# One full tile of the fullest expert worked off between a fused attention/MoE kernel's dense part and its routed loop

## The chip, the cores and the metric

The kernel runs on one core of a Trainium2 chip. The metric is device time in microseconds (us): the time before is the median of 3 runs, and one more execution was taken with the hardware profiler. The core's engines, as the profile names them: PE (TensorE, its weight loads as PEld), DVE (VectorE), ACT (ScalarE), POOL (GpSimd) and SP (SyncE, which here only issues transfers; POOL issues some too).

## The reference

Three stages, all in float32:

```python
kv = einsum('bhsd,bhse->bhde', k, v); out = einsum('bhsd,bhde->bhse', q, kv)      # linear attention, 4 x 8 x 576 x 64
x = rms_norm(out) * g_norm                                                       # then 2304 tokens x 512
# dense mixture: every token through each of 4 experts, weighted by p
for e in range(4): out += p[:, e:e+1] * (maximum(x @ w1[e], 0) @ w2[e])          # 512 -> 1024 -> 512
# routed mixture: each token through one of 8 experts, the best by cosine with expert_emb / tau
for e in range(8): out[idx == e] = gate[idx == e] * (maximum(x[idx == e] @ w1[e], 0) @ w2[e])
```

With the inputs used, the eight routed experts get 120, 639, 189, 727, 149, 36, 293 and 151 tokens, which is 1, 5, 2, 6, 2, 1, 3 and 2 tiles of up to 128 rows: 22 tiles. Of the first 1536 tokens expert 3 gets 484, more than any other.

## The kernel before

Every float32 product is made of three matmuls over operands split into a high and a low part (`three`): high x high, low x high, high x low. ACT makes the high part, DVE or POOL the low one.

**Dense part.** Tokens are worked in thirds of 768 (6 tiles of 128); each third runs 16 steps, 48 in all (k = 0 to 47, `LAST` = 47). A step is `up` (seven block products, written into four PSUM banks and combined by DVE in `combine`) and then `down` for the six tiles of the step before, each added into its rows by a DVE `add` (L965). DVE's list for a step is `combine(k)` and then the six adds; in late steps it also splits the routed experts' weights ahead of time (L973), which SP stores to the DRAM tensor `split_parts`. The last twelve downs stand in an order written out by hand (`TAIL`), with the routing of the last six tiles between them: `flip` (transposes, L1355), `logits` (L1370), `ranks` (L1383 to L1387) on PE; argmax, ranks and slots on DVE; norms on POOL. Blocks of two or three tiles are routed at a time; the first 1536 tokens (12 tiles) are routed and written to their rows by step 38, the last 768 in the tail.

**Dispatch.** POOL's `scatter` (L548) writes each token's row to the DRAM tensor `dispatched_rows`, where each expert has a region. After the last block DVE works out tables of the tiles (L1100 to L1140): which row each tile starts at (`table_row_of_tile`, semaphore `tab_ready` 1), which place in the order of experts it has (`table_place_of_tile`, `tab_ready` 2), and what SP needs to load weights (`tab_ready` 3). A last, partly filled tile of an expert starts further back, and rows that repeat are not stored twice.

**Routed loop.** Tile n: `flip_rows` transposes its rows (L1432), ACT and DVE split them (`rx`, L816 and L1146), `routed_up` makes 24 matmuls, ACT takes the ReLU, `flip_hidden` transposes the hidden rows (L1466), ACT and DVE split them (`rt_parts`, L826 and L1158), `routed_down` makes 24 matmuls, DVE scales by the gate, POOL stores (L608) and loads the rows of a later tile (L594). PE works on up(n+1) before down(n). An expert's split weights are eight pieces of 1 MiB, four for up and four for down; SBUF has two slots, and SP loads the next expert's weights into one while the other is read. A slot's up half is free once the last up of its expert is done, its down half after the last down.

**Between the two.** SP loads the up weights of experts 0 and 1 (L352, eight pieces) once the dense ups are done, then waits for `tab_ready` 1 and all 18 scatters, copies the rows of tiles 0 and 1 (L410), waits until both are there, and loads the down weights of both (L352, eight pieces). The slots of the down weights lie on the dense part's buffers, so they can't be filled before it ends. `load_first` keeps two pieces under way: each waits for the landing of the one before the last. PE runs 48, 8 and 12 matmuls on a unit matrix (L1484, L1487, L1491), whose results nobody reads.

Of the kernel before, what the change touches and what calls it, by code (L numbers as in the profile page):

```python
# [5 lines left out]
F32 = mybir.dt.float32  # L6
# [9 lines left out]
def build(nc, q, k, v, g_norm, probs, w1a, w2a, emb, tau, w1b, w2b, out):  # L16
# [47 lines left out]
    ROUTE_AT = {0: 18, 1: 20, 2: 34, 3: 36}  # L64
    AHEAD_AT = list(range(2, 15)) + [20] + list(range(22, 31)) + [36] + list(range(38, 46))
# [120 lines left out]
    two = keep("two_first", [P, E2])  # L186

# [8 lines left out]
    with ExitStack() as ctx:  # L196
# [28 lines left out]
        filled, scattered = sem("filled"), sem("scattered")  # L225

        part_in = [[sem(f"routed_w{m}_in{c}") for c in range(2)] for m in (1, 2)]
        first_rows_in = [sem("first_rows_in0"), sem("first_rows_in1")]
# [70 lines left out]
        def _(sp):  # L299
# [45 lines left out]
            def load_first(n):  # L345

                e, m, c = n // PCS % 2, n // (2 * PCS), n % PCS
                if n >= 2:

                    e_, m_, c_ = (n - 2) // PCS % 2, (n - 2) // (2 * PCS), (n - 2) % PCS  # L350
                    sp.wait_ge(part_in[m_][c_ % 2], 16 * (e_ * PCS // 2 + c_ // 2 + 1))
                sp.dma_start(W[:, n * PIECE:(n + 1) * PIECE].bitcast(F32),  # L352
                             parts[e, :, (m * PCS + c) * PIECE:(m * PCS + c + 1) * PIECE]).then_inc(part_in[m][c % 2], 16)
# [54 lines left out]
            sp.wait_ge(scattered, 16 * TT)  # L408
            for s in range(2):
                sp.dma_start(xs[:, s, :], rows[bass.ds(first_rows[s], P), :]).then_inc(first_rows_in[s], 16)  # L410

            for s in range(2):
# [24 lines left out]
        def _(pool):  # L437
# [102 lines left out]
            def scatter(b):  # L540

                if b == 0:
                    pool.wait_ge(filled, 32)
                pool.wait_ge(ids_made, BLOCKS[b][0] // TPT + 1)
                pool.wait_ge(slots_ready, b + 1)
                pool.wait_ge(gate_done, b + 1)
                for t in range(*BLOCKS[b]):
                    g.indirect_dma_start(out=rows, out_offset=bass.IndirectOffsetOnAxis(ap=slots[:, t:t + 1], axis=0),  # L548
                                         in_=acc[:, t, :], in_offset=None).then_inc(scattered, 16)
# [40 lines left out]
            pool.wait_ge(scattered, 16 * TT)  # L590

            def load_rows(kk, s):
                r = pool.value_load(tab_r[0:1, bass.ds(kk, 1)], min_val=0, max_val=E2 * CAP + P)
                pool.dma_start(xs[:, s, :], rows[bass.ds(r, P), :]).then_inc(rows_in[s], 16)  # L594


            for s in range(2):

                pool.wait_ge(rx_done, s + 1)
                pool.wait_ge(gi_copied, s + 1)  # L600
                load_rows(s + 2, s)
# [10 lines left out]
            with pool.Fori(0, PAIRS) as i:  # L612
# [13 lines left out]
        def _(act):  # L626
# [179 lines left out]
            for t in range(TT - TPT, TT):  # L806
# [4 lines left out]
            exponentials(NB - 1)  # L811


            def rx(n, s):
                act.wait_ge(rx_done, n + 1)
                A(rxh[:, s, :], ps[:, 7 * s, :], ACT.Copy).then_inc(rx_hi, 1)  # L816

            def relu_rows(n):
                for half in range(2):
                    act.wait_ge(rh_done, 2 * n + half + 2)  # L820
                    A(hs[:, half * 512:(half + 1) * 512], ps[:, 1 + half, :], ACT.Relu).then_inc(rh_relu, 1)

            def rt_parts(n, s):
                for half in range(2):
                    act.wait_ge(rt_done, 2 * n + half + 1)
                    A(rhh[:, s, half * 512:(half + 1) * 512], ps[:, 3 + half, :], ACT.Copy).then_inc(rt_hi, 1)  # L826


            for s in range(2):
                act.wait_ge(s_out[s], 32 * (NAHEAD // 2))  # L830
            act.wait_ge(tab_ready, 2)
            tiles = act.value_load(tab_n[0:1, 0:1], min_val=TT, max_val=KT)
            rx(0, 0)
            rx(1, 1)
            relu_rows(0)
            rt_parts(0, 0)
            with act.Fori(0, PAIRS) as i:
# [16 lines left out]
        def _(dve):  # L854
# [190 lines left out]

            for k in range(STEPS):
                t = k // NU
                if k % NU == 0 and k:
# [23 lines left out]
            for n, (kk, j) in enumerate(TAIL):  # L1072
                add(kk, j)
                if n == 7:
# [30 lines left out]
            step(V.tensor_scalar(ec(5), ec(1), float(-P), float(CAP), ALU.mult, ALU.add), False)  # L1105
# [14 lines left out]
            step(V.scalar_tensor_tensor(kc_(5), kc_(3), float(P), kc_(0), ALU.mult, ALU.add))  # L1120
# [5 lines left out]
            step(V.tensor_copy(tab_n[:, 0:1], ec(2)[:, E2 - 1:E2]), False)  # L1126
# [13 lines left out]
            V.tensor_copy(tab_c[:, :], ec(8)).then_inc(tab_ready, 1)  # L1140
            dve.wait_ge(tab_ready, 3)


            def rx(n, s):
                dve.wait_ge(rx_hi, n + 1)
# [396 lines left out]
```

## Time and profile before

| | us |
|---|---|
| median of 3 runs | 1151.87 (1150.92 to 1154.58) |
| the profiled execution's own time | 1151.53 |
| span of its profile | 1149.9 |

| engine | busy, share of the span |
|---|---|
| PE | 1125.5 us, 98% |
| DVE | 728.5 us, 63% |
| POOL | 655.9 us, 57% |
| ACT | 455.3 us, 40% |

Some 1.6 us of the execution's time lie outside the span. PE is busy nearly always, but part of what it does in the middle is the unread matmuls, so its busy share is not its useful share. All times in rows below are microseconds from the span's start; a mean or a duration is given in ns where a column says so.

### The profile page before, as it was taken

To read this page: it belongs to the slowest core of one execution; us is meant where nothing else is said; L and a number is where in the kernel's file an instruction comes from. 1 tells how busy PE (TensorE), PEld (TensorE's weight loads), DVE (VectorE), ACT (ScalarE), POOL (GpSimd) and SP (SyncE) were. 2 spreads that over 40 slices of the span, in tenths; PEclk is the share of its full clock that TensorE was granted. 3 is DMA by queue.
4 is the path that set the end of the run, shared out by engine and by line. 5 is a ranking of instruction groups with operands and counts; after the bars stand their busy time and mean duration, and the time that the engine had idled before them with its cause. 6 is when DMAs were issued, how large, how long until landed. Compare 5 with 4: busy or idle time off the path is not lost.

```text
span 1149.9 us, 18699 instructions
## 1 busy us (share of the span) xinstructions
PE 1125.5 (98%) x6206; PEld 992.3 (86%) x6207; DVE 728.5 (63%) x1159; ACT 455.3 (40%) x808; POOL 655.9 (57%) x609
## 2 busy tenths in 40 slices
PE   8999999999999999999999999999999999999996
PEld 8888889999889888998889888998887788888885
DVE  4877888888976788888875878888662222222221
ACT  4773444444434444444434444444222222222220
POOL 1587777799867777899867777777330111111101
PEclk9999999999999999999999999999989999999998
DMA  9955777777512448877612448777369749427960
GB/s 245 268 157 180 267 268 271 278 275 276 199 45 78 142 131 302 289 278 261 216 37 75 137 146 302 279 273 270 144 243 383 273 183 372 153 100 302 374 238 13
DMA packets 102433, 250.87 MB, mean 218 GB/s; under 512 B 8254, under 2 KB 48190, under 8 KB 94171
## 3 DMA queue, kind: packets, MB, share of 16 engines
q1 hardware_dynamic: 97360, 235.18, 59.2%
q0 software_dynamic: 4800, 14.72, 3.7%
q8 instruction: 41, 0.67, 0.2%
q14 instruction: 29, 0.24, 0.1%
q10 hardware_dynamic: 203, 0.05, 0.0%
HBM read 170.99 MB, written 79.98 MB: 218 GB/s over the span
## 4 chain that ended last, share of the span: by engine, by line
PE 82%; DVE 7%; POOL 4%; issue 3%; DMA 2%; ACT 2%; SPq 0%; DVEq 0%; POOLq 0%; ACTq 0%
PE ps L1277 25%; PE ps L1279 25%; PE ps L1278 25%; PE ps L1466 2%; DMA w_raw<-in_moe_w_dram 1%; DVE x_rows L965 1%; POOL w_lo L483 1%; PE ps L1235 1%; PE ps L1432 1%; PE ps L1370 1%; DVE hT_lo L954 1%; PE ps L1205 1%; DVE attn_rows L887 1%; DVE x_ops_lo L978 1%; DVE hT_lo L952 0%
## 5 line engine op out<-in xcount | busy, mean ns | idle before, releaser
L1277 PE MATMUL ps<-x_ops_hi,w_hi 128*128 128x384 f32 x672 | 226.5, 337 | 3.4 <-DVE sum L935 3.2
L1277 PE MATMUL ps<-w_hi,hT_hi 128*128 128x512 f32 x576 | 227.1, 394 | 0.4
L1279 PE MATMUL ps<-x_ops_hi,w_lo 128*128 128x384 f32 x672 | 225.7, 336 | 0.0
L1279 PE MATMUL ps<-w_hi,hT_lo 128*128 128x512 f32 x576 | 225.4, 391 | 0.0
L1278 PE MATMUL ps<-x_ops_lo,w_hi 128*128 128x384 f32 x672 | 225.2, 335 | 0.0
L1278 PE MATMUL ps<-w_lo,hT_hi 128*128 128x512 f32 x576 | 225.0, 391 | 0.0
L965 DVE SCALAR_TENSOR_TENSOR x_rows<-ps,dense_probs,x_rows 128x512 f32<-128x512 f32 x270 | 189.8, 738 | 22.2 <-PE ps L1279 22.2
L608 POOL DMA_INDIRECT out_dram<-y_rows,row_ids x22 | 22.6, 1026 | 237.3 <-DVE y_rows L1168 141.9
L492 POOL TENSOR_TENSOR w_lo<-w_raw,w_hi 128x512 fp32r<-128x512 f32 x96 | 149.5, 1577 | 8.0 <-ACT w_hi L702 8.0
L1158 DVE TENSOR_TENSOR rhT_lo<-ps,rhT_hi 128x512 fp32r<-128x512 f32 x44 | 28.4, 686 | 172.9 <-ACT rhT_hi L826 172.9
L478 POOL TENSOR_TENSOR w_lo<-w_raw,w_hi 128x512 fp32r<-128x512 f32 x48 | 62.2, 1295 | 126.7 <-ACT w_hi L690 126.6
L1277 PEld LDWEIGHTS ps<-x_ops_hi,w_hi 128*128 128x128 f32 x672 | 126.1, 188 | 8.8 <-DVE sum L935 5.3
L728 ACT ACTIVATE product<-ps 128x384 f32<-128x384 f32 x48 | 23.6, 491 | 265.8 <-PE ps L1279 265.7
L1279 PEld LDWEIGHTS ps<-w_hi,hT_lo 128*128 128x128 f32 x576 | 108.1, 188 | 22.9
L1278 PEld LDWEIGHTS ps<-x_ops_lo,w_hi 128*128 128x128 f32 x672 | 126.2, 188 | 1.8
L1277 PEld LDWEIGHTS ps<-w_hi,hT_hi 128*128 128x128 f32 x576 | 108.2, 188 | 21.2 <-DVE x_rows L965 0.9
L1279 PEld LDWEIGHTS ps<-x_ops_hi,w_lo 128*128 128x128 f32 x672 | 126.1, 188 | 0.0
L1278 PEld LDWEIGHTS ps<-w_lo,hT_hi 128*128 128x128 f32 x576 | 108.2, 188 | 20.6
L483 POOL TENSOR_TENSOR w_lo<-w_sums,w_hi 128x512 fp32r<-128x512 f32 x96 | 122.2, 1294 | 0.7 <-ACT w_hi L678 0.7
L973 DVE TENSOR_TENSOR ahead_lo<-ahead_raw,ahead_hi 128x1024 fp32r<-128x1024 f32 x64 | 84.0, 1312 | 1.3 <-ACT ahead_hi L753 1.3
L1277 PE MATMUL ps<-w_slots,rxT_hi 128*128 x176 | 71.3, 405 | 1.1 <-issue 1.1
L954 DVE SCALAR_TENSOR_TENSOR hT_lo<-sum,hT_hi 128x384 fp32r<-128x384 f32 x48 | 71.7, 1493 | 0.5
(198 smaller groups left out, 2006.8 us busy)
## 6 DMA issues: line engine op xcount, KB each, us to landing
w_slots<-split_parts SPq DMA_DIRECT2D x64, 1024.0 KB, 5.6
w_raw<-in_moe_w_dram SPq DMA_DIRECT2D x96, 512.0 KB, 3.5
ahead_raw<-in_moe_w_dram SPq DMA_DIRECT2D x64, 512.0 KB, 6.6
split_parts<-ahead_hi SPq DMA_DIRECT2D x64, 512.0 KB, 4.4
split_parts<-ahead_lo SPq DMA_DIRECT2D x64, 512.0 KB, 5.8
row_tile<-dispatched_rows POOLq DMA_DIRECT2D x20, 257.0 KB, 5.8
kv<-in_k_dram SPq DMA_DIRECT2D x16, 288.0 KB, 7.9
kv<-in_v_dram SPq DMA_DIRECT2D x16, 288.0 KB, 8.2
```

The lines of the kernel that those rows point to most:

```text
L478: g.tensor_tensor(w1l[s][:, 0:2], w1_raw4[:, :, :, 0:P], w1h[s][:, 0:2].bitcast(F32), ALU.subtract)
L483: last = g.tensor_tensor(w1l[s][:, 3 + m:5 + m].rearrange("p m c n -> p (m c n)"), tsum[:, m:m + 2].rearrange("p m c n -> p (m c n)"), w1h ...
L492: last = g.tensor_tensor(w2l[s][:, c, :], w2raw[:, c, :], w2h[s][:, c, :].bitcast(F32), ALU.subtract)
L728: A(p1[:, :], ps[:, 0, 0:HT], ACT.Copy).then_inc(p1_copied, 1)
L954: V.scalar_tensor_tensor(hl[s][:, 1, 0:HT], u2[:, :], 0.0, hh[s][:, 1, 0:HT].bitcast(F32), ALU.max, ALU.subtract).then_inc(h_lo, 1)
L965: V.scalar_tensor_tensor(acc[:, t, 0:D], ps[:, 4 + n % 4, :], pr[:, t, e:e + 1], acc[:, t, 0:D], ALU.mult, ALU.add).then_inc(y_used, 1)
L973: V.tensor_tensor(slo[:, s, :], sraw[:, s, :], shi[:, s, :].bitcast(F32), ALU.subtract).then_inc(s_lo, 1)
L1158: V.tensor_tensor(rhl[:, s, half * 512:(half + 1) * 512], ps[:, 3 + half, :], rhh[:, s, half * 512:(half + 1) * 512].bitcast(F32), ALU.sub ...
L1277: mm(out_, ah, bh, start=(first and m == 0), stop=False, skip_group_check=not final or not first)
L1278: mm(out_, ah, bl, start=False, stop=False, skip_group_check=not final or not first)
L1279: last = mm(out_, al, bh, start=False, stop=(final and m == n - 1), skip_group_check=not final or not first)
L1466: last = tr(ps[:, 3 + half, c * P:(c + 1) * P], hs[:, m:m + P], ident[:, :])
```

## The change

One tile, the "star", is the first 128 rows of the expert that has most of the first 1536 tokens. It is worked through before the tables of all tiles are there.

- DVE picks that expert at the start of step 41 (`choose_star`, 13 small operations): its number and its region's start for SP, and numbers by which the tables later leave the star's rows out.
- SP reads the two numbers, copies the star's rows before the dense ups end, loads the star's up weights (slot 1) and then expert 0's up weights (slot 0, four pieces). After the last dense down it loads the star's down weights. Then come the rows of the next two tiles, and behind them twelve pieces: expert 1's up, expert 0's down, expert 1's down. The star's loads (`load_early`) don't wait for one another, and the wait for the landing of the rows ahead of the weights is gone.
- PE transposes the star's rows in the tail, behind the second of its twelve downs. The star's up and down are dealt out in pieces between the last logits and the first tile of the loop; the unread matmuls are gone.
- ACT and DVE split for it; DVE's two halves of the split hidden rows stand inside the calculation of the tables.
- Tiles are numbered anew: the star is tile 0, the 21 others follow. The number of tiles stays 22. The first pair of the loop is written out.

```diff
+    STAR_AT = 41
+            def load_early(m):
+                for c in range(PCS):
+                    n = (2 * m + 1) * PCS + c
+                    sp.dma_start(W[:, n * PIECE:(n + 1) * PIECE].bitcast(F32),
+                                 parts[e_star, :, (m * PCS + c) * PIECE:(m * PCS + c + 1) * PIECE]).then_inc(early_in[m][c // 2], 16)
...
-            sp.wait_ge(up_done, OPS * STEPS)
+            sp.wait_ge(star_ready, 1)
+            e_star = sp.value_load(tab_s[0:1, 0:1], min_val=0, max_val=E2 - 1)
+            r_star = sp.value_load(tab_s[0:1, 1:2], min_val=P, max_val=E2 * CAP)
...
-            for n in range(2 * PCS):
-                load_first(n)
+            sp.wait_ge(scattered, 16 * T0)
+            sp.dma_start(xs[:, 0, :], rows[bass.ds(r_star, P), :]).then_inc(first_rows_in[0], 16)
+            sp.wait_ge(up_done, OPS * STEPS)
+            load_early(0)
+            load_first(0, 0)
...
+            load_early(1)
             sp.wait_ge(tab_ready, 1)
...
-            for s in range(2):
-                sp.wait_ge(first_rows_in[s], 16)
-            for n in range(2 * PCS, 4 * PCS):
-                load_first(n)
+            sp.wait_ge(rh_done, 3)
+            load_first(1, 0)
+            load_first(0, 1)
+            sp.wait_ge(ry_done, 2)
+            load_first(1, 1)
...
+                if k == STAR_AT:
+                    choose_star()
...
                 add(kk, j)
+                if n == 2:
+                    rx(0, 0)
+                    V.tensor_copy(early_gi[:, :], xs[:, 0, D:D + 2]).then_inc(gi_copied, 1)
...
+            rt_half(0, 0, 0)
             step(V.tensor_tensor_scan(ec(4), unit[:, :], ec(3), 0.0, ALU.mult, ALU.add))
...
             V.tensor_scalar(tab_o[:, :], kc_(1), kcu(2), None, ALU.min).then_inc(tab_ready, 1)
+            rt_half(0, 0, 1)
...
             logits(TT - 1, LAST)
+            early_up(0, (0, 1, 2))
             ranks(NB - 1, LAST)
+            early_up(0, (3,))
+            early_up(1, (0, 1))
+            pe.wait_ge(rank_read, NB)
+            flip_half(0, 0)
+            early_up(1, (2, 3))
+            early_down((0, 1))
+            flip_half(0, 1)
+            early_down((2, 3))
+            early_down((4, 5))
...
-            for _ in range(2 * WARM):
-                mm(ps[:, 6, 0:P], ident[:, :], ident[:, :], start=True, stop=True)
             pe.wait_ge(tab_ready, 2)
...
             flip_rows(1, 1)
-            routed_up(0, 0)
-            flip_hidden(0)
-            with pe.Fori(0, PAIRS) as i:
+            early_down((6, 7))
+            flip_rows(2, 0)
+            routed_up(1, 1)
+            flip_hidden(1)
+            flip_rows(3, 1)
+            routed_up(2, 0)
...
+            routed_down(1, 1, 0, e, off)
+            flip_hidden(2)
+            routed_down(1, 1, 1, e, off)
+            with pe.Fori(1, PAIRS) as i:
```

SP's list from the end of the dense ups on. Of before, from the wait for `up_done` (L352 is a weight piece, L407 reads a row number into a register, L410 copies rows):

```order
L352 DMA w_slots<-split_parts 128x2048 [waits ahead_out1,ahead_out0,up_done]
L352 DMA w_slots<-split_parts 128x2048
...
L407 TENSOR_LOAD table_row_of_tile [waits w2_split,tab_ready,y_done,h_lo]
...
L410 ISA [waits scattered]
L410 DMA row_tile<-dispatched_rows 128x514
...
L352 DMA w_slots<-split_parts 128x2048 [waits routed_w1_in0,first_rows_in1,first_rows_in0]
L352 DMA w_slots<-split_parts 128x2048 [waits routed_w1_in1]
L352 DMA w_slots<-split_parts 128x2048 [waits routed_w2_in0]
```

And of the changed kernel (L368 is a piece of the star's weights, L361 a piece of another expert's, L432 and L433 copy rows):

```order
L368 ISA [waits w2_split,y_done,h_lo]
L368 DMA w_slots<-split_parts 128x2048
...
L429 TENSOR_LOAD table_row_of_tile [waits tab_ready]
...
L432 ISA [waits scattered_late,scattered]
L432 DMA row_tile<-dispatched_rows 128x514
L433 ISA
L433 DMA row_tile<-dispatched_rows 128x514
L361 DMA w_slots<-split_parts 128x2048 [waits routed_w1_in0,rh_done]
L361 DMA w_slots<-split_parts 128x2048 [waits routed_w1_in1]
```

Four weight pieces now stand ahead of the table's read and the rows' copies, and twelve behind them, where eight stood.

PE's list behind the last logits. Of before (L1383 to L1387 are the last ranks, L1484 to L1491 the unread matmuls, L1432 the transposes of rows):

```order
L1370 MATMUL ps<-enT,xt_route 128x8 [waits c12_done,xt_copied]
...
L1383 MATMUL ps<-r_oh,tri 128x16 [waits rank_read,c21_done,oh_ready]
L1385 MATMUL ps<-r_oh,ones 128x8
L1387 MATMUL ps<-r_oh,ones 128x8 x2
L1484 MATMUL ps<-ident 128x128 x24
L1487 MATMUL ps<-ident 128x128 [waits tab_ready]
```

And of the changed kernel (L1354 is the first matmul of three, L1462 the last ranks, L1518 the transposes of hidden rows, L1496 those of rows):

```order
L1354 MATMUL ps<-w_slots,rxT_hi 128x512 [waits early_w1_in0,y_used,rx_split]
...
L1462 MATMUL ps<-r_oh,tri 128x16 [waits rank_read,c21_done,oh_ready]
...
L1354 MATMUL ps<-w_slots,rxT_hi 128x512 [waits lg_read,early_w1_in0,y_used,rx_split]
...
L1518 MATMUL ps<-ident,h_rows 128x128 [waits rh_relu,rank_read]
...
L1354 MATMUL ps<-w_slots,rhT_hi 128x512 [waits early_w2_in0,rt_split]
...
L1354 MATMUL ps<-w_slots,rhT_hi 128x512 [waits early_w2_in1,rt_split]
...
L1496 MATMUL ps<-ident,row_tile 128x128 [waits first_rows_in1]
```

Nine of the star's matmuls stand ahead of the last ranks, and 33 more between these and the first transposes of the loop's rows; each part has a wait of its own.

## Rows read from the trace of the kernel before

**Rows 1.** The page: each engine's busy time, share of the span, instructions.
```profile
PE 1125.5 (98%) x6206; PEld 992.3 (86%) x6207; DVE 728.5 (63%) x1159; ACT 455.3 (40%) x808; POOL 655.9 (57%) x609
```

**Rows 2.** The chain of waits between dense and routed part: start, length, what.
```profile
846.12 0.33 issue
...
856.47 0.47 SPq L407
...
858.00 2.64 DMA row_tile<-dispatched_rows
860.68 0.66 PE ps L1432 x4
...
863.16 0.50 PE ps L1277
```

**Rows 3.** The timeline of PE there: start, length, instruction, idle time before it.
```profile
850.72 0.19 PE L1383 MATMUL ps<-r_oh,tri 128*128 128x16 bf16 x1 [1.82 <-DVE r_oh L1021]
...
850.85 8.33 PE L1484 MATMUL ps<-ident 128*128 128x128 f32 x48
```

**Rows 4.** The timeline of PE in the routed part's first tiles.
```profile
871.59 0.50 PE L1277 MATMUL ps<-w_slots,rxT_hi 128*128 x1 [0.54 <-issue]
...
883.78 0.60 PE L1432 MATMUL ps<-ident,row_tile 128*128 128x128 f32 x4
...
896.30 0.60 PE L1432 MATMUL ps<-ident,row_tile 128*128 128x128 f32 x4
```

**Rows 5.** The timeline of DVE at step 41 and in the routing.
```profile
725.22 0.56 DVE L935 TENSOR_TENSOR sum<-ps,product 128x384 f32<-128x384 f32 x1 [0.88 <-PE ps L1279]
...
727.23 0.56 DVE L937 TENSOR_TENSOR sum<-ps,product 128x384 f32<-128x384 f32 x1 [1.45 <-PE ps L1279]
...
849.67 0.17 DVE L1017 TENSOR_REDUCE r_cols<-r_logit 128x2 f32<-128x16 f32 x1
849.87 0.17 DVE L1018 TENSOR_TENSOR r_eq<-r_logit,r_cols 128x16 f32<-128x16 f32 x1
...
854.68 0.40 DVE L1116 TENSOR_TENSOR r_cmpd<-r_cmpd,expert_cols 128x240 f32<-128x240 f32 x1
```

**Rows 6.** The chain of waits in the tail: four transposes on PE.
```profile
833.10 0.44 PE ps L1355 x4
```

**Rows 7.** The page, costliest groups: the split of hidden rows, mean ns of one.
```profile
L1158 DVE TENSOR_TENSOR rhT_lo<-ps,rhT_hi 128x512 fp32r<-128x512 f32 x44 | 28.4, 686 | 172.9 <-ACT rhT_hi L826 172.9
```

**Rows 8.** The timeline of SP: start, length, weight pieces issued.
```profile
823.54 5.16 SPq L352 DMA_DIRECT2D w_slots<-split_parts  x3
...
837.01 5.29 SPq L352 DMA_DIRECT2D w_slots<-split_parts  x3
...
861.46 0.81 SPq L352 DMA_DIRECT2D w_slots<-split_parts  x2
866.27 0.33 SPq L352 DMA_DIRECT2D w_slots<-split_parts  x1
868.93 0.33 SPq L352 DMA_DIRECT2D w_slots<-split_parts  x1
...
884.58 3.10 SPq L397 DMA_DIRECT2D w_slots<-split_parts  x2
```

**Rows 9.** The timeline of POOL: the last scatter.
```profile
854.30 0.96 POOL L548 DMA_INDIRECT dispatched_rows<-x_rows,slots  x1 [0.30 <-issue]
```

**Rows 10.** All scatters (L548): from issue to landing.
```profile
DMA to landing us min/median/max: 2.9/6.7/10.7
```

**Rows 11.** All of POOL's copies of rows (L594), made while weights load.
```profile
DMA to landing us min/median/max: 2.9/5.8/9.3
```

**Rows 12.** Stretches: busy of PE, PEld, DVE, ACT, POOL, then PEclk, DMA share, GB/s.
```profile
845.00:850.00 5.00, 3.50 (x31) 3.03 (x29) 3.07 (x17) 2.18 (x8) 2.65 (x5) 0.97 0.49 199
850.00:855.00 5.00, 4.28 (x23) 4.28 (x24) 4.31 (x25) 0.60 (x4) 3.66 (x4) 0.50 0.38 144
855.00:860.00 5.00, 5.00 (x39) 4.88 (x37) 3.88 (x21) 0.00 (x0) 0.26 (x1) 0.84 0.37 111
```

More of the change, by code:

```diff
@@ L186, in build @@
     two = keep("two_first", [P, E2])
+    star = keep("star", [P, E2])
+    star_col = keep("star_cols", [P, 3])
+    jumps = keep("region_jumps", [P, E2])
+    kstart = keep("tile_ends", [P, TAB])
+    tab_s = keep("table_star", [P, 2], I32)
+    early_gi = keep("early_gate_and_id", [P, 2])
     tab_o = keep("table_place_of_tile", [P, TAB], I32)
@@ L589, in _, with load_rows @@
             pool.wait_ge(tab_ready, 1)
-            pool.wait_ge(scattered, 16 * TT)
-            def load_rows(kk, s):
-                r = pool.value_load(tab_r[0:1, bass.ds(kk, 1)], min_val=0, max_val=E2 * CAP + P)
+            pool.wait_ge(scattered, 16 * T0)
+            pool.wait_ge(scattered_late, 16 * TPT)
+            def load_rows(n, s):
+                r = pool.value_load(tab_r[0:1, bass.ds(n - 1, 1)], min_val=0, max_val=E2 * CAP + P)
                 pool.dma_start(xs[:, s, :], rows[bass.ds(r, P), :]).then_inc(rows_in[s], 16)
[L597 to L601, printed above, removed]
+            pool.wait_ge(rx_done, 2)
+            pool.wait_ge(gi_copied, 2)
+            load_rows(3, 1)
             pool.wait_ge(tab_ready, 2)
@@ L610, in store @@
                                      bounds_check=NTOK - 1, oob_is_err=False).then_inc(stored[s], 16)
-            with pool.Fori(0, PAIRS) as i:
+            for s in range(2):
+                store(s, s)
+                pool.wait_ge(rx_done, s + 3)
+                pool.wait_ge(gi_copied, s + 3)
+                load_rows(s + 4, s)
+            with pool.Fori(1, PAIRS) as i:
                 with pool.If(2 * i < tiles):
@@ L805, in _, with rx, relu_half, rt_half @@
                         exponentials(b)
-            for t in range(TT - TPT, TT):
+            def rx(n, s):
+                act.wait_ge(rx_done, n + 1)
+                A(rxh[:, s, :], ps[:, 7 * s, :], ACT.Copy).then_inc(rx_hi, 1)
+            def relu_half(n, half):
+                act.wait_ge(rh_done, 2 * n + half + 2)
+                A(hs[:, half * 512:(half + 1) * 512], ps[:, 1 + half, :], ACT.Relu).then_inc(rh_relu, 1)
+            def rt_half(n, s, half):
+                act.wait_ge(rt_done, 2 * n + half + 1)
+                A(rhh[:, s, half * 512:(half + 1) * 512], ps[:, 3 + half, :], ACT.Copy).then_inc(rt_hi, 1)
+            def relu_rows(n):
+                for half in range(2):
+                    relu_half(n, half)
+            def rt_parts(n, s):
+                for half in range(2):
+                    rt_half(n, s, half)
+            for s in range(2):
+                act.wait_ge(s_out[s], 32 * (NAHEAD // 2))
+            rx(0, 0)
+            for t in range(T0, TT):
                 route(t)
@@ L811, in _ @@
             exponentials(NB - 1)
[L814 to L830, printed above, removed]
+            for half in range(2):
+                relu_half(0, half)
+                rt_half(0, 0, half)
             act.wait_ge(tab_ready, 2)
             tiles = act.value_load(tab_n[0:1, 0:1], min_val=TT, max_val=KT)
-            rx(0, 0)
             rx(1, 1)
-            relu_rows(0)
-            rt_parts(0, 0)
-            with act.Fori(0, PAIRS) as i:
+            rx(2, 0)
+            relu_rows(1)
+            rt_parts(1, 1)
+            rx(3, 1)
+            relu_rows(2)
+            rt_parts(2, 0)
+            with act.Fori(1, PAIRS) as i:
                 with act.If(2 * i < tiles):
@@ L1461, in flip_hidden @@
                 for half in range(2):
-                    pe.wait_ge(rh_relu, 2 * n + half + 1)
-                    for c in range(4):
-                        m = half * 512 + c * P
-                        last = tr(ps[:, 3 + half, c * P:(c + 1) * P], hs[:, m:m + P], ident[:, :])
-                    last.then_inc(rt_done, 1)
+                    flip_half(n, half)
             def routed_down(n, s, wh, e, off):
@@ L1480, in routed_down @@
                     last.then_inc(ry_done, 1)
[L1483 to L1484 removed]
             pe.wait_ge(tab_ready, 2)
[L1486 to L1487 removed]
             tiles = pe.value_load(tab_n[0:1, 0:1], min_val=TT, max_val=KT)
[L1489 to L1491 removed]
             flip_rows(1, 1)
[L1493 to L1495 removed]
+            early_down((6, 7))
[4 more added lines that the diff above has]
+            routed_up(2, 0)
+            e = place_of(1)
+            off = pe.snap((e % 2) * (2 * WCOL))
+            routed_down(1, 1, 0, e, off)
+            flip_hidden(2)
+            routed_down(1, 1, 1, e, off)
+            with pe.Fori(1, PAIRS) as i:
                 with pe.If(2 * i < tiles):
```

158 lines of the change are left out of this document (108 added, 50 removed).

## The prediction, written before the changed kernel ran

> **What bounds the kernel now.** I read the page's busy shares first. PE is busy 98% of the span [rows 1], so time can only come out where PE works for nothing. The timeline of the stretches shows where that is: behind the dense part, in 850 to 855, ACT has 0.6 us of work and PE's clock is granted at 0.50 [rows 12]; what fills PE there is 48 unread matmuls, 8.33 us of them, behind an idle wait of 1.82 us [rows 3]. The chain of waits confirms it: the last dense matmul has ended by 846.12, and then a chain of small things (norms on POOL, argmax, ranks and tables on DVE, two register reads by SP, the copy of the rows) ends with the first transposes of rows at 860.68 and the first routed matmul at 863.16 [rows 2]. That is a hole of 17.0 us in which PE has only a few small routing matmuls. From there on the routed part is PE's alone: from 883.78 to 896.30, one tile, 12.52 us [rows 4], and 22 tiles of it.
>
> So the most that moving one tile into the hole can give is 12.5 us, if nothing that ends the hole is made later. The sum is what comes off that.
>
> I fix one point and compare it in both kernels: the transposes at 896.30, when the downs of tiles 0 and 1 and the ups of tiles 0, 1 and 2 are done [rows 4]. In the changed kernel the same point has been reached when the star, tile 1 and the up of tile 2 are done; behind it the same 20 downs follow, the same experts in the same order (expert 3 with one tile less), the same last pair. Whatever this point gains, the end gains.
>
> **The dense part gets longer: 1.5 + 0.45 us.** `choose_star` is 13 small operations on DVE at the start of step 41. Such operations follow each other at 0.20 us (849.67, 849.87) [rows 5], so 2.6 us. DVE stood idle 0.88 us before this step's first sum at 725.22 [rows 5]; the sum comes 1.7 us late, PE's fourth product waits for it and has some 0.3 us to spare (the next sum, which waits for that product, starts 2.0 us later at 727.23, so a product takes 1.0; beside it runs the sum of 0.56 us and its semaphore). The step gets 1.5 us longer; PE bounds the dense part, so nothing gives it back. Bounds: 0, if DVE catches up, and 2.6. The star's row transposes are four on PE in the tail; four such took 0.44 us [rows 6]. DVE's split there (0.69 us like its neighbours [rows 7]) and its copy lie beside the downs, since PE has four banks; without that cover, 0.9 us. The early copy of the star's rows and SP's register reads lie under step 41 to 47.
>
> **The routing chain: 0.25 + 0.7 us.** Nine of the star's up matmuls stand ahead of the last ranks, at 0.233 us each (24 ups and 12 downs are the 8.5 us from 871.59 to the flips before 883.78, [rows 4]) 2.1 us, where PE was idle for 1.82 us [rows 3]: the ranks come 0.25 us later. One half of the star's hidden split stands in DVE's tables ahead of `tab_ready` 1: 0.69 us [rows 7]; the operation ahead of it was at 854.68 [rows 5], now 857, and the star's hidden rows are transposed and copied by ACT by 856.5, so it adds no wait. If they are late it would, by as much as they are: bounds 0.7 and 2. The second half stands behind `tab_ready` 2, ahead of nothing that the rows wait for. The register reads, at 856.47 before [rows 2], start at 859.4, and the rows could be issued at 860.9 instead of 858.00.
>
> **The scatters now share the DMA engines.** Before, no weights moved from about 848 to 861: DMA share 0.38 and 0.37 [rows 12]. Now four pieces, the star's down weights, are issued at 847.4, when the last down is done. Eight pieces took from 823.54 to about 847 (the eighth issued at 841.97, the end of its row less 0.33, and landed some 5 us later, as the first did), 2.9 us each [rows 8]; the four and the four scatters in the hole keep the engines busy until 861 to 863. The last scatter, issued at 854.30 before [rows 9], is issued at 856.5. Its landing takes 2.9 to 10.7, median 6.7 [rows 10]; before, it was there within 3.7 us (rows issued at 858.00 [rows 2]). I take 6.0, as the weights run out around then: landed 862.5, so that the rows wait for the scatter, not for the table. Bounds: 860.9 (the table's) and 867.2.
> The Trainium skill (DMA: Bandwidth & Descriptors, "Queues, rings and completion order") says that each DMA engine goes round-robin between queues, a packet at a time, so a scatter from POOL's queue isn't behind all of SP's weights, but behind a packet of them each time. By that the delay for six scatters would be bounded by the four pieces and the date would be no later than mine; the trace's median of 6.7 against 2.9 for the quietest fits, and the sum would not change.
>
> **When PE starts the loop.** Rows issued 862.5, landed after 2.64 [rows 2], 865.2; transposes 0.66 [rows 2], the star's last six matmuls 1.4, transposes 0.44, a register read 0.5 [rows 4]: first routed matmul at 868.5, against 863.16. The star's other 42 matmuls fit before: the last logits end at 850.72 less 1.82 [rows 3], now 850.85, and from there they need 9.8 us plus two transposes of 0.44 us, and even with the waits for ReLU, splits and the last two weight pieces (862.5) they are done at 864. From the first routed matmul to the point it was 8.43 us to 871.59 and 12.19 to 883.78 for one up, transposes, the next up and a whole down [rows 4]. So PE alone would be at the point at 868.5 + 20.6 = 889.1, 7.2 us earlier than 896.30.
>
> **But the weights are not there.** Before, a first pair of pieces was issued at 861.46, the first landed at 866.27 (the third issue waits for it), and the eighth at 887.4 (second issue of the row at 884.58) [rows 8]: 4.8 us and then 3.0 each. PE wanted the first four from 877.3 on (a flip and 24 matmuls, 6.5 us, before 883.78) and the others only from 889.8. Now the pieces start behind the rows, at 863.4, and the rows' two copies go first, 0.3 us net: landings at 868.5, and 3.0 on each. The order is expert 1's up (1 to 4), expert 0's down (5 to 8), expert 1's down. PE reaches up(2) at 876.9: piece 4 lands at 877.5, in time for its second half. It reaches the first half of down(1) at 882.5: piece 6 lands at 883.5, a wait of 1.0. It reaches the second half at 887.2: piece 8 lands at 889.5, a wait of 2.3. Then 12 matmuls, 2.8 us: the point is at 892.3. Piece 12 lands at 901.5, PE wants it at 902. So the point moves from 896.30 to 892.3: 4.0 us. In the sum: 12.5 moved, less 1.95 dense, 0.95 routing chain, 1.6 for the scatter, 0.85 for PE's start behind the rows, 3.2 for the weights.
>
> Profiled 1151.53 less 4.0 is 1147.5. The profiled execution lies 0.34 below the median, so the forecast is 1147.9.
>
> **Rivals.**
> - *The weights keep up* (1144.7). If a piece takes 2.6 us, or the rows start at 860.9 and the pieces with them, PE's own 889.1 (or 887.5) rules. For it: the first two landed 2.66 apart (866.27, 868.93). Against: 26 us for eight pieces in this very place [rows 8]. 0.2.
> - *PE's clock is down while the star is worked* (1149.5). The clock was granted at 0.97 in 845 to 850 and 0.50 in 850 to 855, so 1.2 instead of 2.4 GHz, after a stretch in which PE did transposes and small logits and was idle, and it was 0.84 in 855 to 860 with PE busy throughout [rows 12]. If it still falls where it fell, the nine matmuls ahead of the last ranks take 4.2 us instead of 2.1, and table and scatter come 1.9 later, of which the later scatter finds emptier queues: 1.6 net. If it falls only behind 862, the wait for weights hides it. Against: now dense matmuls follow the last logits at once. 0.15. The Trainium skill (TensorE: Matmul & The Clock Gate, "Part 1: The HAM clock gate") says that throttled is the default and activity releases it; the trace agrees (0.50 to 0.84 under the unread matmuls). By that rule the star's own matmuls would have to warm the clock.
> - *The dispatch starves under the weights* (1155.7, slower). The scatter takes 10.7 us [rows 10], landing at 867.2, and the rows' copy, too, runs under traffic at 9.3, the slowest of POOL's copies [rows 11], instead of 2.64. Rows at 876.7, PE starts at 879.7, the point is at 900.3: 4.0 late. It decides once rows land behind 873 (then PE's start, 3 us later, plus 20.6 passes 896.30). Against: the four pieces run out by 863, and nothing is issued between them and the rows. 0.12.
> - *The change doesn't do what it says* (1151.5): the star's parts don't fit, because weights for its down land at 868 or later and six or eighteen matmuls wait there, ahead of the loop. 0.08.
>
> **How the numbers follow.** The forecast's case has 0.45; its own range, from the stall of step 41 (0 to 2.6) and the start of the pieces (861.8 to 866), is 1145.5 to 1150. A measurement of this kernel can tell 0.3%, 3.5 us: faster is below 1148.4, slower above 1155.3. Faster: 0.32 of the 0.45, the 0.2, and a little of the clock's case, 0.54. Slower: most of the starving case, with larger sizes too, and a tail of the others, 0.11. The rest, 0.35, is within. Range 1143.5 to 1153: it leaves out most of the starving case and the fastest corner of the first rival.
>
> **What would show it.** Step 41 longer by 1.5 us, the sum at 725.22 late by 1.7. No row of unread matmuls; star matmuls from about 850.8, the clock in 850 to 860 at 1.00. The last scatter landing about 862.5, rows issued just behind, first routed matmul near 868.5. Two waits of PE in down(1) that end with weights, 1.0 and 2.3 us; none after that. 12.5 us per tile as before. Wrong it would be if the pieces land closer than 3.0 apart, if PE waits for the star's down weights or a split for more than 2 us, or if the clock is at 0.50 ahead of the last ranks.

## The result, and the profile after

The changed kernel takes 1160.54 us (median of 5, 1159.96 to 1162.53) against 1151.56 in the same comparison: 1.0077 times, 95% interval 1.0061 to 1.0093. It is 0.77% slower where I forecast 0.3% faster. Its span in the profile is 1158.5, 8.6 longer.

I compare the two traces at the first sum of `combine`, which stands once in each step. DVE's timeline of the changed kernel around step 41 answers to [rows 5] (start, length, instruction, idle time before it):

```profile
725.62 0.15 DVE L1087 TENSOR_TENSOR expert_cols<-next_row,region_base 128x8 f32<-128x8 f32 x1
...
726.99 0.15 DVE L1094 TENSOR_SCALAR table_star<-star_cols 128x1 int32<-128x1 f32 x1
727.06 1.13 DVE L1096 TENSOR_SCALAR region_jumps<-star 128x8 f32<-128x8 f32 x1
728.23 0.65 DVE L1097 SCALAR_TENSOR_TENSOR region_jumps<-star,region_jumps 128x7 f32<-128x7 f32 x1
728.91 1.18 DVE L1098 SCALAR_TENSOR_TENSOR region_base<-star,region_base 128x8 f32<-128x8 f32 x1
730.13 0.15 DVE L1099 TENSOR_SCALAR star_cols<-star 128x1 f32<-128x1 f32 x1
730.32 1.01 DVE L1100 TENSOR_SCALAR tile_ends<-k_numbers,star_cols 128x30 f32<-128x30 f32 x1
731.37 0.56 DVE L973 TENSOR_TENSOR sum<-ps,product 128x384 f32<-128x384 f32 x1
```

POOL's timeline of the same kernel there:

```profile
726.89 1.28 POOL L502 TENSOR_TENSOR w_lo<-w_raw,w_hi 128x512 fp32r<-128x512 f32 x1 [3.60 <-ACT w_hi L717]
728.13 0.73 POOL L503 TENSOR_TENSOR w_lo<-w_raw,w_hi 128x256 fp32r<-128x256 f32 x1
728.81 2.48 POOL L507 TENSOR_TENSOR w_lo<-w_sums,w_hi 128x512 fp32r<-128x512 f32 x2
```

The first eight operations follow each other at some 0.2 us, as forecast. From 726.89 POOL works, and four of the next five end together with an operation of POOL: 728.19 and 728.17, 728.88 and 728.86, 730.09 and the first of the two of L507 (some 730.05, if each takes half of the 2.48 us), 731.33 and 731.29. The fifth (L1099, one column, one operand) takes 0.15 us. The sum stands at 731.37; before it was at 725.22. PE's timeline and its stretch show what hung on it (columns of the stretch as in [rows 12]):

```profile
731.98 0.44 PE L1354 MATMUL ps<-x_ops_hi,w_hi 128*128 128x384 f32 x1 [4.49 <-DVE sum L973]
```

```profile
731.00:733.00 2.00, 1.02 (x4) 1.02 (x5) 0.89 (x2) 0.00 (x0) 2.00 (x3) 0.86 0.41 125
733.00:735.00 2.00, 2.00 (x8) 2.00 (x8) 1.05 (x2) 0.00 (x0) 0.98 (x2) 0.50 0.70 222
735.00:737.00 2.00, 2.00 (x11) 2.00 (x10) 0.64 (x3) 0.90 (x2) 1.92 (x4) 0.78 0.73 251
```

PE stood for 4.5 us, and behind that its clock was granted at 0.50, 1.2 GHz. What the step costs is read from the first sums of step 40 and step 42, first in the kernel before:

```profile
709.69 0.56 DVE L935 TENSOR_TENSOR sum<-ps,product 128x384 f32<-128x384 f32 x1 [1.17 <-PE ps L1279]
...
740.75 0.56 DVE L935 TENSOR_TENSOR sum<-ps,product 128x384 f32<-128x384 f32 x1 [0.39 <-PE ps L1279]
```

and in the changed kernel:

```profile
711.05 0.56 DVE L973 TENSOR_TENSOR sum<-ps,product 128x384 f32<-128x384 f32 x1 [1.27 <-PE ps L1356]
...
748.42 0.56 DVE L973 TENSOR_TENSOR sum<-ps,product 128x384 f32<-128x384 f32 x1 [1.45 <-PE ps L1356]
```

In step 40 they are 1.36 us apart (that much comes from the attention part and differs from profile to profile), in step 42, and still in step 47, 7.7. So step 41 costs 6.3 us: 4.5 of waiting, and the other 1.8 is the slow clock's as far as the three rows of the stretch tell: 0.14, 0.50 and 0.22 below the full clock over 2 us each are 1.7 us.

Behind the dense part, the chain of waits of the changed kernel answers to [rows 2] (start, length, what):

```profile
854.95 0.66 PE ps L1434 x4
...
861.80 0.96 POOL dispatched_rows L572
862.75 0.30 issue
863.06 8.87 DMA dispatched_rows<-x_rows,slots
872.13 0.33 SPq L432
872.65 0.33 SPq L433
873.08 0.38 SPq L361
873.51 7.19 DMA w_slots<-split_parts
...
894.65 6.25 DMA w_slots<-split_parts
900.92 6.81 DMA w_slots<-split_parts
907.75 7.49 DMA w_slots<-split_parts
```

It is a chain of transfers: the last scatter, then the pieces. PE's waits in its timeline, against [rows 4] (879.10 is the first routed matmul of the loop):

```profile
871.47 0.47 PE L1354 MATMUL ps<-w_slots,rhT_hi 128*128 128x512 f32 x1 [3.43 <-DMA w_slots<-split_parts]
...
879.10 0.55 PE L1354 MATMUL ps<-w_slots,rxT_hi 128*128 x1
...
894.95 0.50 PE L1354 MATMUL ps<-w_slots,rhT_hi 128*128 x1 [2.36 <-DMA w_slots<-split_parts]
...
901.14 0.50 PE L1354 MATMUL ps<-w_slots,rhT_hi 128*128 x1 [0.69 <-DMA w_slots<-split_parts]
...
904.04 0.60 PE L1496 MATMUL ps<-ident,row_tile 128*128 128x128 f32 x4
```

The last row is the point that I compare (896.30 before). The last tile's flip of the dense part waits until 854.95; before, it stood at 846.46 (the 0.33 us at 846.12 in [rows 2] are part of that wait):

```profile
846.46 0.66 PE L1355 MATMUL ps<-ident,x_rows 128*128 128x128 f32 x4 [0.41 <-DVE x_rows L965]
```

So the 8.6 us are: 1.4 in the attention part, 6.3 in step 41, 0.8 in the tail; then 49.1 us to the point instead of 49.8, 0.75 back; and 0.9 behind it, where PE once more waited for a piece (1.56 us at 915.48). The tile moved into the hole brought 0.75 us, and a wait behind the point took it away.

### The profile page after: what moved, and what is told of

It reads as the page before. It is cut to its first block, busy times and chain, and to the rows that moved or that the text cites. A ratio compares the mean times of both kernels' runs of the same rounds, so it can differ in the third digit from the quotient of the medians.

```text
span 1158.5 us, 18470 instructions
## 1 busy us (share of the span) xinstructions
PE 1121.4 (97%) x6138; PEld 985.6 (85%) x6139; DVE 730.5 (63%) x1172; ACT 455.4 (39%) x808; POOL 653.9 (56%) x608
## 4 chain that ended last, share of the span: by engine, by line
PE 78%; DMA 7%; DVE 6%; POOL 4%; issue 3%; ACT 1%; SPq 1%; ACTq 0%; POOLq 0%; DVEq 0%
PE ps L1354 24%; PE ps L1356 24%; PE ps L1355 24%; DMA w_slots<-split_parts 4%; DMA w_raw<-in_moe_w_dram 1%; PE ps L1518 1%; DVE x_rows L1003 1%; POOL w_lo L507 1%; PE ps L1312 1%; PE ps L1449 1%; DMA q<-in_q_dram 1%; DMA dispatched_rows<-x_rows,slots 1%; PE ps L1496 1%; DMA probs_rows<-in_moe_domain_probs_dram 1%; DVE hT_lo L992 1%
## 5 line engine op out<-in xcount | busy, mean ns | idle before, releaser
L1354 PE MATMUL ps<-x_ops_hi,w_hi 128*128 128x384 f32 x672 | 227.5, 338 | 7.8 <-DVE sum L973 7.6
L1354 PE MATMUL ps<-w_hi,hT_hi 128*128 128x512 f32 x576 | 227.2, 394 | 0.1
L1354 PEld LDWEIGHTS ps<-x_ops_hi,w_hi 128*128 128x128 f32 x672 | 126.6, 188 | 13.3 <-DVE sum L973 9.9
L1354 PEld LDWEIGHTS ps<-w_hi,hT_hi 128*128 128x128 f32 x576 | 108.3, 188 | 20.7
L507 POOL TENSOR_TENSOR w_lo<-w_sums,w_hi 128x512 fp32r<-128x512 f32 x96 | 122.3, 1295 | 0.8 <-ACT w_hi L705 0.8
L1354 PE MATMUL ps<-w_slots,rhT_hi 128*128 (+1 forms) x176 | 72.8, 414 | 8.8 <-DMA w_slots<-split_parts 8.0
L1354 PE MATMUL ps<-w_slots,rxT_hi 128*128 (+1 forms) x176 | 71.5, 407 | 0.0
```

Source lines behind the costliest of these rows:

```text
L507: last = g.tensor_tensor(w1l[s][:, 3 + m:5 + m].rearrange("p m c n -> p (m c n)"), tsum[:, m:m + 2].rearrange("p m c n -> p (m c n)"), w1h ...
L1354: mm(out_, ah, bh, start=(first and m == 0), stop=False, skip_group_check=not final or not first)
```

## The experiments

Medians stand beside those of the kernel before in the same comparison; the ratio has its 95% interval. It isn't the quotient of the two medians and differs from it by up to 0.11%; where I give a difference by the ratios, it is the ratio's.

**b_star: the kernel before and the 13 operations alone.**

```diff
+                if k == 41:
+                    choose_star()      # the 13 operations, into tiles that nobody reads
```


> The kernel before with the 13 small DVE operations alone, at the start of step 41, their results unused. Theory (a DVE operation of this kind that meets a running POOL operation stands until that one ends): eight operations of 0.2 us and then four of 0.65 to 1.2 us, DVE's next sum 6.2 us after it would have been, PE waits 4.5 us, its clock falls to 0.50 for some 4 us, and the whole is 6.3 us slower than before. Rival (13 operations of 0.2 us cost what I forecast, the other 4.8 us came with another part of the change): 1.5 us slower.

Measured: 1158.63 against 1152.21, ratio 1.0054 (1.0037 to 1.0071), 6.4 us slower by the medians, 6.2 by the ratio. The trace repeats the changed kernel's:

```profile
726.46 0.96 DVE L1065 TENSOR_SCALAR region_jumps<-star 128x8 f32<-128x8 f32 x1
727.46 0.65 DVE L1066 SCALAR_TENSOR_TENSOR region_jumps<-star,region_jumps 128x7 f32<-128x7 f32 x1
728.14 1.19 DVE L1067 SCALAR_TENSOR_TENSOR base_unused<-star,region_base 128x8 f32<-128x8 f32 x1
729.36 0.15 DVE L1068 TENSOR_SCALAR star_cols<-star 128x1 f32<-128x1 f32 x1
729.55 1.01 DVE L1069 TENSOR_SCALAR tile_ends<-k_numbers,star_cols 128x30 f32<-128x30 f32 x1
```

PE waits 4.49 us for the sum here, too. Steps 40 and 41 together take 7.0 us longer in this profile, as the clock already falls during that wait (0.50 from 730 to 736). The loss of the step is the 13 operations'; no other part of the change is needed for it. b_col, b_wide and b_two ask what in them waits.

**b_col: 12 of the 13 with one operand of one column.**

```diff
+                step(V.tensor_tensor(ecol[:, 0, 0:1], run[:, 0:1], ebase[:, 0:1], ALU.subtract))
+                for n in range(12):
+                    step(V.tensor_scalar(<star_col, one column>, <star_col, the other column>, 1.0, 1.0, ALU.add, ALU.mult))
```


> The kernel before with 13 DVE operations at the start of step 41 as well, but each on one column, 12 of them with a single SBUF operand; their results are unused. Theory (what waits for POOL is an operation with two SBUF operands or a wide one with one operand; the one of a single column in the changed kernel took 0.15 us in the middle of the waiting ones): 0.2 us each, 2.6 in all, no fall of the clock, 1.5 us slower than before. Rival (every DVE operation waits while POOL works): 6 us slower, as with the real ones.

Measured: 1154.50 against 1152.21, ratio 1.0009 (0.9993 to 1.0025), so 1.0 us slower by the ratio, with room for 1.5. From the first sum of step 40 to that of step 41 it is 17.04 us instead of 15.53: the 1.5 us of my forecast, with the same number of operations at the same place. The first row is the eleven last, the second is POOL at work beside some six of them (they end at 729.23):

```profile
727.19 2.04 DVE L1058 TENSOR_SCALAR star_cols<-star_cols 128x1 f32<-128x1 f32 x11
```

```profile
728.09 1.28 POOL L484 TENSOR_TENSOR w_lo<-w_raw,w_hi 128x512 fp32r<-128x512 f32 x1 [3.60 <-ACT w_hi L696]
```

**b_wide: the 12 with one operand of eight columns.** The edit is that of b_col with tiles of eight columns.

> As b_col (the kernel before with 13 unused DVE operations at the start of step 41), but 12 of them take one operand of eight columns. Theory (a wide operation with one SBUF operand waits for the end of the POOL operation that runs): those that meet POOL's six operations each stand until one ends, 8 us in all, PE waits some 7 us, the clock falls, 8 us or more slower than before. Rival (only operations with two SBUF operands wait): 1.5 us slower, as b_col.

Measured: 1161.15 against 1152.08, ratio 1.0078 (1.0060 to 1.0097), 9 us slower. POOL starts on an operation of 1.28 us at 726.01 here; the operation of 726.18 ends at 727.32, POOL's at 727.29:

```profile
725.97 0.18 DVE L1058 TENSOR_SCALAR region_jumps<-star 128x8 f32<-128x8 f32 x1
726.18 1.14 DVE L1058 TENSOR_SCALAR star<-region_jumps 128x8 f32<-128x8 f32 x1
```

**b_two: all 13 with two operands of one column.**

```diff
-                    step(V.tensor_scalar(...))
+                    step(V.tensor_tensor(<one column>, <the other column>, ebase[:, 1:2], ALU.add))
```


> As b_col, but all 13 take two SBUF operands of one column. Theory (two SBUF operands wait, whatever their width): as b_wide, 8 us or more slower than before. Rival (only the width counts): 1.5 us slower, as b_col.

Measured: 1161.79 against 1152.08, ratio 1.0080 (1.0062 to 1.0098), 9 us slower. The eleven last, beside six operations of POOL:

```profile
726.57 7.68 DVE L1058 TENSOR_TENSOR star_cols<-star_cols,region_base 128x1 f32<-128x1 f32 x11
```

Both forms wait, each rival falls: a wide operation with one SBUF operand and a narrow one with two. Only one operand of one column got through. The Trainium skill (SBUF — State Buffer, "SBUF: two separate sides") says that a port pair is shared by DVE and GpSimd under an exclusive lock held for a whole instruction, and that DVE takes it for operations in a two-port performance mode or, against a GpSimd operation that reads SBUF, with two SBUF inputs. The traces agree for two inputs (0.65 and 1.18 us in the changed kernel for operations that take 0.17 where POOL is idle, in a_late). That the operation of eight columns ran in such a mode no row shows; it waited like the others.

**a_late: the choice moved to step 46, behind its first add.**

```diff
-    STAR_AT = 41
+    STAR_AT = 46
...
-                if k == STAR_AT:
-                    choose_star()
...
+                        if k == STAR_AT and j == 0:
+                            choose_star()
```


> The changed kernel with the 13 operations moved from the start of step 41 to behind the first add of step 46, where POOL is idle and DVE has no weights to split. Theory (step 41 made 6.3 us of the loss and nothing behind it gives that back): 6.3 us faster than the changed kernel, 2.5 us slower than before, dense part's end within 1 us of before plus 0.45. Rival (the dispatch is bound by something that doesn't shift with the dense end): 0 to 3 us faster than the changed kernel.

Measured: 1152.82 against 1152.21, ratio 1.0002 (0.9987 to 1.0018), 0.75% less than the changed kernel's ratio, and 0.2 us slower than before where I had expected 2.5 (the interval ends at 2.1). The operations that took 1.13 and 0.65 us take 0.16 and 0.17 now, as POOL is idle, and the one of 1.18 takes 0.17:

```profile
813.43 0.16 DVE L1096 TENSOR_SCALAR region_jumps<-star 128x8 f32<-128x8 f32 x1
813.63 0.17 DVE L1097 SCALAR_TENSOR_TENSOR region_jumps<-star,region_jumps 128x7 f32<-128x7 f32 x1
```

It came back by 8.6 us rather than 6.3 by the ratios, more than the step; their intervals (1.8 us each way) leave room for that, and the profile's span is just 6.9 us shorter, 1.2 of them in the attention part. What is left is a kernel as fast as before, with the tile moved. In this profile it is 50.9 us from the last flip (848.06) to the point (898.94), where the kernel before took 49.8 and the changed one 49.1. Where did the tile's 12.5 us go?

**a_nodown: the star's down weights not loaded.**

```diff
-            load_early(1)
...
-                pe.wait_ge(early_in[1][half], 32)
+                for c in range(2):
+                    pe.wait_ge(part_in[0][c], 32)
...
-                    m = 6 * WCOL + half * 2 * PIECE + c % (FCH // 2) * D
+                    m = half * 2 * PIECE + c % (FCH // 2) * D
```


> The same as the last, and the star's down weights are left out: its down matmuls read expert 0's up weights instead, so the star's 128 rows of the output are not the reference's. No weight traffic lies beside the last scatters. Theory (the scatter took 8.9 us because four weight pieces shared the DMA engines): scatter landed within 4 us of its issue, rows issued 5 us earlier, no wait of PE for the star's weights, the twelve pieces start 5 us earlier; some 5 us faster than a_late, 2.5 us faster than before. Rival (the scatters are slow because DVE's work on the tables now keeps POOL from writing descriptors): scatter still 7 us or more, 0 to 1 us faster than a_late.

Measured: 1151.51 against 1152.21, ratio 0.9989 (0.9972 to 1.0006). On the scatter the theory held, with DVE's work on the tables beside it as in a_late, so the rival falls: issued at 858.78, its rows followed 4.1 us later. In a_late it was 8.8:

```profile
856.18 8.57 DMA dispatched_rows<-x_rows,slots
864.95 0.33 SPq L432
```

and here SP's rows stand in the chain of waits behind its register reads and no scatter:

```profile
861.54 0.28 SPq L428
862.11 0.27 SPq L428
862.86 0.34 SPq L431
```

On the time it failed: 1.5 us by the ratios instead of 5. PE waits for the pieces behind the rows (5.2 us in three waits; in a_late 4.7 for the same ones), and in this profile its clock fell in front of the last ranks (a matmul of 512 columns every 0.43 us from 852.04 on), the rival of the forecast, which put the last scatter 9.5 us behind the last flip instead of 8.1. So a second bound lay behind the scatter; how much of the missing 3.5 us is the clock's isn't shown.

**a_pace: half of the star's down weights behind the rows, all 24 pieces kept.**

```diff
-            load_early(1)
+            load_early(1, range(2))
...
+            load_early(1, range(2, 4))          # behind the rows' copies
...
-            early_down((4, 5))
             flip_rows(1, 1)                     # with what stands between left out
+            early_down((4, 5))
             early_down((6, 7))
```


> a_late (star chosen at run time, all 24 pieces) with the second half of the star's down weights loaded behind the rows, and its last twelve matmuls behind the transposes of tile 1's rows. Theory (in this version the stream of pieces bounds the start: it only changes places with the scatters): rows 3 us earlier, but 14 pieces behind them instead of 12, PE waits 4 us or more for the star's weights, within 1.5 us of a_late. Rival (the late scatter bounds): 2 to 3 us faster than a_late.

Measured: 1152.99 against 1151.85, ratio 1.0014 (1.0002 to 1.0027). By the ratios it is 1.4 us slower than a_late, within the 1.5 that I had expected. The rows are issued at 861.76, 4.7 us behind the last scatter, and it doesn't help, as PE then waits for the star's last pieces:

```profile
872.30 0.77 PE L1355 MATMUL ps<-w_slots,rhT_hi 128*128 128x512 f32 x1 [7.13 <-DMA w_slots<-split_parts]
```

In this version the stream of pieces bounds; the scatter and the pieces change places in it.

**f_one: the star's weights stay.** The star is always expert 1, which relies on it having at least 128 of the first 1536 tokens.

```diff
-                step(V.tensor_reduce(star_col[:, 1:2], ecol[:, 1, :], AX.X, ALU.min))
+                step(V.tensor_scalar(star_col[:, 1:2], star_col[:, 0:1], 0.0, float(1 - E2), ALU.mult, ALU.add))
...
-            load_early(0)
             load_first(0, 0)
+            load_first(1, 0)
...
-            sp.wait_ge(rh_done, 3)
-            load_first(1, 0)
             load_first(0, 1)
-            sp.wait_ge(ry_done, 2)
-            load_first(1, 1)
...
```

(What is left out are the waits on these pieces, set to match.)

> a_late with expert 1 always taken as the star (it has 417 of the first 1536 tokens here; the kernel relies on that), whose weights then stay in slot 1 for its other tiles: eight of the 24 pieces of the start fall away, and behind the rows come four (expert 0's down) and not twelve. Theory (what the moved tile gains in a_late is paid back by PE's waits for pieces behind the rows, some 4.7 us there): those waits are under 1 us, 4 to 5 us faster than a_late and than before, about 1148. Rival (the hole itself, with the late scatter and rows, takes as long with the star as without): within 1.5 us of a_late.

Measured: 1147.33 against 1151.85, ratio 0.9959 (0.9945 to 0.9973), 0.41% faster than before. The list of a_late's waits has 7.8 us of PE's for weights, 3.1 of them for the star's; here one of 3.2 is left, the star's. The moved tile is one of expert 1 instead of expert 3, so the order of the tiles behind it differs, too; the rival (within 1.5 us of a_late) falls all the same.

**f_hide: f_one, and the star's last weights hidden.**

```diff
-            load_early(1)
+            load_early(1, range(2))
...
+            load_early(1, range(2, 4))          # behind the rows' copies
...
-            first_results()                     # DVE: scales the star's result
             rx(2, 0)
             gates(2, 0)
+            first_results()
...
-            early_down((4, 5))
...
             flip_rows(1, 1)
-            early_down((6, 7))
             flip_rows(2, 0)
             routed_up(1, 1)
+            early_down((4, 5))
+            early_down((6, 7))
```


> f_one, and the second half of the star's down weights is loaded behind the rows, the star's last twelve matmuls standing behind the up of tile 1. Theory (scatters are slow beside weight traffic, and rows wait for the last one): with two pieces instead of four beside them, which are there before the last two scatters are issued, the last scatter lands within 5 us instead of 8.6, the rows are issued 3 us earlier, PE's wait of 3.1 us for the star's weights is gone; 2 to 3 us faster than f_one, about 1145.5. Rival (the scatter's time is not the pieces' doing): the last scatter still takes 8 us, within 1 us of f_one or slower.

Measured: 1145.22 against 1151.85, ratio 0.9938 (0.9925 to 0.9951): 7.1 us by the ratio, faster than both kernels, and 2.4 us faster than f_one by the ratios, as expected. POOL and SP:

```profile
861.01 0.96 POOL L575 DMA_INDIRECT dispatched_rows<-x_rows,slots  x1 [0.30 <-issue]
```

```profile
865.45 0.33 SPq L432 DMA_DIRECT2D row_tile<-dispatched_rows  x1
```

4.4 us from scatter to rows where f_one had 8.8 (857.69 to 866.49). Other than I had expected, the two early pieces were not there before the last scatters; they landed when PE's wait for them ended, 2.6 us behind the last scatter's issue:

```profile
863.71 0.47 PE L1357 MATMUL ps<-w_slots,rhT_hi 128*128 128x512 f32 x1 [1.89 <-DMA w_slots<-split_parts]
```

PE's waits for pieces are down to 2.1 us.

**f_41: f_hide with the choice back at the start of step 41.** The edit is that of a_late, undone.

> f_hide with the 13 operations that choose the star back at the start of step 41, as in the changed kernel. Theory (the loss of step 41 and the gain behind the dense part are independent): 6.3 us slower than f_hide, 1151.5, the same as before. Rival (part of it is taken up in the hole): 3 to 4 us slower than f_hide.

Measured: 1151.64 against 1152.08, ratio 0.9998 (0.9987 to 1.0009), 0.60% or 6.9 us more than f_hide by the ratios. The rival's 3 to 4 us fall: within these intervals the loss in step 41 and the gain behind the dense part are independent.

## Why the prediction was wrong

The profile is 8.6 us longer where I had it 4.0 shorter. Of these 12.6 us, 1.4 are the attention part's; 4.8 and 0.3 are the dense part's, 5.2 the hole's up to the point, 0.9 what lay behind it.

- **The dense part gets longer: 1.95.** This is the step that failed by most. The slack (0.88 us of DVE's idle time) and the number of operations were right; their pace was taken from operations at 849.67 [rows 5], which met no running POOL operation, and at step 41 they do. The term measured 6.3 us, not 1.5, outside my own bound of 2.6; b_star shows it alone, and b_col shows that operations that don't wait would have cost the 1.5. The tail added 0.8 instead of 0.45. The trace of before had rows of the wait: a low-part operation with two SBUF operands (L954) took 0.54 us in one step, when POOL was idle, and 1.65 in the next, when POOL was at work until 717.65:

```profile
701.61 0.54 DVE L954 SCALAR_TENSOR_TENSOR hT_lo<-sum,hT_hi 128x384 fp32r<-128x384 f32 x1
...
716.42 1.65 DVE L954 SCALAR_TENSOR_TENSOR hT_lo<-sum,hT_hi 128x384 fp32r<-128x384 f32 x1
```

- **The routing chain: 0.95.** Right: the last scatter was issued 8.1 us behind the last flip, as forecast, and the table of rows was written 0.86 us later behind it than before.
- **The scatters share the DMA engines.** The mechanism was right, the term mis-sized: the last scatter landed 8.87 us behind its issue instead of 6.0 (at most 4.1 with no piece beside it in a_nodown, 4.4 with two in f_hide), so the rows were issued 17.2 us behind the last flip instead of 14.1. That is 3.1 of the 5.2 us. The star's last pieces landed at 871.4, 16.5 us behind the flip where I had 14.1, and PE waited 3.4 us that I had not: more than the 2 us that I had named as a sign of being wrong. In the three profiles with four pieces beside it (this one, a_late, f_one) the scatter landed some 0.5 us behind the last of them (871.4 and 871.93 here): in effect it waited for nearly all of them, and they ran 2.4 us longer than I had put them. So the date was later than mine, where my argument from the round robin had it no later. It came near the starving rival's 10.7; alone (4.0 less 3.1) it would not have made the kernel slower.
- **But the weights are not there.** Right in kind: waits of 2.36 and 0.69 us for expert 0's down, forecast 1.0 and 2.3. The eighth piece landed 28.0 us behind the first's issue, forecast 26.1: 1.9 of the 5.2. The twelfth made a wait of 1.56 us that I had put at nothing, so that the end didn't gain what the point gained. f_one shows what this bound is worth: eight pieces fewer, 0.43% less than a_late.
- **PE's clock.** It was at 1.00 from 846 to 872, so the star ran at 2.4 GHz but for its last matmuls, and it fell to 0.50 in 873 to 879, behind PE's wait for the star's last weights. The waits for weights at 894.95 and 901.14 came after it; that they took up what it cost, as that rival has it, follows from the pieces landing when they did, but no run shows it. a_nodown's profile shows that it can fall ahead of the ranks, too.
- **Slips in the sums.** The terms of PE's start add up to 868.1, not 868.5, and the starving rival's point at 900.3 gives 1155.9, not 1155.7. Neither changes the forecast, as the weights set its point.

The first failure made the kernel clearly slower than before; scatter and pieces took the gain. Without the first (a_late) the change is level, since these two take all or nearly all that the moved tile brings.

## What to carry to other kernels

Before small DVE operations are put into a dense stretch, look at what POOL does in that microsecond: with two SBUF operands, or a single one of eight columns, each stood until POOL's operation ended. Eleven of one column took 2.04 us with one operand and 7.68 with two. Work moved into a hole brings its operands' transfers with it, and these compete with the ones that end the hole; count the bytes from the start of the hole to the first point of steady work, in both versions. Here the early tile paid once its weights were ones that stay (f_one).

## What the runs showed of the hardware that I had not expected

- DVE operations of 0.15 to 0.24 us took 0.65 to 1.19 us and ended within 0.04 us of POOL's running operation (a subtraction of two SBUF tiles). One SBUF operand of eight columns or two operands of one column are enough (b_wide, b_two); one operand of one column isn't (b_col), and neither were the sums that read PSUM (0.56 us at 731.37, with POOL at work from 731.25). Beside POOL's scatter at 850.00, 1.04 us long, operations with two SBUF operands took their 0.17 us (850.08 and 850.49 before).
- A wait of 4.5 us in the middle of dense matmuls was followed by a granted clock of 0.50, and the step lost some 1.8 us more (2.5 in b_star's profile). A wait of 2.16 us was, too (a_nodown: matmuls again from 881.49, 0.50 in 883 to 886).
- A scatter of 128 rows (257 KB) from POOL's queue landed within 4.1 us of its issue with no pieces of 1 MiB on SP's queue, within 4.4 to 4.7 with two of them (f_hide, a_pace, f_41; in f_hide the last of the two landed 2.6 us behind that issue), and took 8.6 to 8.9 beside four.
